# Splitting weights and tables inside the recurrence on GpSimd, and handing the first batch's rows over within the last step

## The chip, the cores and the metric

One core of one Trainium2 chip. The metric is device time in microseconds (us), the median of three runs. Engines: TensorE (PE), VectorE (DVE), ScalarE (ACT), GpSimd (POOL), and SyncE (SP), whose queue issues every DMA of this kernel.

## The reference, cut to what matters

Three layers follow each other, for 4 batches, 768 tokens and 8 heads of 40 columns (320 in all).

```
# 1 recurrence, per batch and head, over t = 0..767
y[t]  = r[t] @ state
Sa    = state @ a[t]
state = state * w[t] - outer(Sa, b[t]) + outer(v[t], k[t])
# 2 gated unit: x is y as [4, 768, 320]
h = relu(x @ w_in)                 # 320 -> 1024
g = sigmoid(conv3(h))              # three taps along the tokens
x = (h * g) @ w_out                # 1024 -> 320
# 3 Fourier mixing and a channel layer
u = x + real(fft2(x)); un = normalise(u)
out = u + relu(un @ w_ch1) @ w_ch2 # 320 -> 1280 -> 320
```

## The kernel before, in words

The kernel is two blocks of engine programs, `attention` (layer 1) and `channels` (layers 2 and 3). At the end of a block all engines meet at a barrier.

**attention.** The 768 tokens are taken in 6 steps (`STEPS`) of 128, each of two chunks of 64 (`c` = 0, 1). `attention_jobs` writes one list of jobs by hand, and each engine walks the list in that order and does its own part of each job: (stage, step g, chunk c, batch b). In step g the list does the sequential part of step g ("sat", "sa", "st", "xn", "y", "xt") beside the preparation of step g+1 (the triangular inverse by substitution, "sub", on VectorE) and of step g+2 ("scan", "at", "keys", "gram"). So a step is a column of decays (`w`) that is loaded into the tile `w_in`, scanned forward and backward on VectorE (L407, L412), and multiplied into a, k and b on GpSimd (L350, L358). GpSimd also scales the state (L365, stage "xn") and copies diagonal blocks of the inverse (L376, stage "diag"), which the jobs "pu" (TensorE, L685) wait for. SP walks the same list: it loads w for step g+1 right after the last scan of step g (L266), keys at "tb" (L280), r and v after "y" (L259, L260), and it stores y to a DRAM scratch (L318, 8 DMAs a step, rows of 128 numbers). SP is in order: each wait holds all that stands behind it.

The weights of layer 2, `w1` and `w2`, are needed in two fp32r parts, a rounded high part and the remainder. In the last step SP loads them raw (L325, five DMAs, after the last "pu"), ACT makes the high parts (L524) and VectorE the low parts (L433). SP then stores the last y and waits for all of it (L328) before the barrier.

**channels.** SP loads batch 0's rows from the DRAM scratch (L889, L891), ACT and VectorE split them (L969, L1108), and TensorE starts with `first_up` (L1291). Per batch there are 8 columns f: `first_up` (relu on ACT, L1009), the convolution (ACT L1015, VectorE L1194 and L1196), the sigmoid (ACT L1023), the gate (VectorE L1206, L1207), its split (ACT L984, VectorE L1118), and `first_down` (TensorE L1315). Then the transform (L1369 to L1384), the normalisation (L1166 to L1173), the GpSimd copy of a tail (L944), and the channel layer (L1291, L1349). From batch 1 on the channel layer of the batch before runs between these. Beside batch 0, the tables of the transform and the weights `w3` and `w4` come in 11 pieces through the tile `raw`: SP loads (L908), ACT makes the high part in `take_pieces` (L961), and GpSimd the low part (L937).

Of the kernel before, what the change touches and what calls it, by code (L numbers as in the profile page):

```python
# [19 lines left out]
DM = NH * D  # L20
# [12 lines left out]
FIRST_PIECES = 5  # L33


def attention_jobs():
# [31 lines left out]

    def kind(g, k):
        return [("gram", g, k, i) for i in range(NB)]  # L70
# [3 lines left out]
    order = each("scan", 0) + one("at", 0) + each("decays", 0) + each("keys", 0) + one("ends", 0)  # L74
# [3 lines left out]
    order += one("at", 1) + each("decays", 1) + each("keys", 1) + one("ends", 1)  # L78
    for g in range(STEPS):
        if g + 1 < STEPS:  # L80
# [15 lines left out]
            last = grams(g + 2, (1,))  # L96
            order += grams(g + 2, (0,)) + last[:2]
            order += merge(g + 1, last[2:], each("xt", g, 1, 2)) + each("decays", g + 2) + one("split", g + 2) + subs(g + 2, 0, SUBS[0])
        else:

            order += [(stage, g, 0, b) for stage in ("sat", "sa", "st") for b in range(2 if stage == "sat" else NB)]
            rest = each("xn", g, 0) + each("y", g, 0) + each("xt", g, 0, 2)
            rest += each("sat", g, 1, 2) + each("sa", g, 1) + each("st", g, 1)
            order += interleave(rest, [("table", g, 0, i) for i in range(FIRST_PIECES)])
            order += each("y", g, 1)
# [3 lines left out]
NOT_PSUM = ("scan", "at", "decays", "keys", "ends", "eye", "table", "split", "sub", "unsplit", "diag")  # L109


def first_tables(nc, ctx, dram):
# [8 lines left out]
    raw = sb("first_raw", [128, 3 * FF + NF * DM])  # L121
    pieces = []
    for t in range(3):
        cols = slice(t * FF, (t + 1) * FF)
        pieces.append((dram["w1"][:, cols], raw[:, cols], w1[:, 0, t, :], w1[:, 1, t, :]))
    n = NF * DM // 2
    parts = [w2[:, k, :, :].rearrange("p f d -> p (f d)") for k in range(2)]
    for t in range(2):
        cols = slice(t * n, (t + 1) * n)
        pieces.append((dram["w2"][:, cols], raw[:, 3 * FF + t * n:3 * FF + (t + 1) * n], parts[0][:, cols], parts[1][:, cols]))  # L130
    return w1, w2, pieces


def attention(nc, ctx, dram, tables, kept):
# [44 lines left out]
    ident, conv = kept  # L179
# [32 lines left out]

    s_piece = [sem(f"s_piece{i}") for i in range(FIRST_PIECES)]
    s_high = sem("s_high")
    s_low = sem("s_low_a")
    s_y = [sem(f"s_y{i}") for i in range(NB)]
# [33 lines left out]
    w1, w2, w_pieces = tables  # L250
# [3 lines left out]
    def _(sp):  # L254
# [6 lines left out]

        def load_w(g):
# [24 lines left out]

        load_w(0)
# [11 lines left out]
        for stage, g, c, b in order:  # L300
            more = g + 1 < STEPS
            if stage == "scan" and b == NB - 1 and more:
                load_w(g + 1)
# [1263 lines left out]
```

## Time and profile before

| what | value |
|---|---|
| median of 3 runs | 980.86 us (976.91 to 984.75) |
| profiled execution, its own time | 991.84 us |
| its span, first to last instruction | 990.0 us |
| PE busy | 860.3 us (87%) |
| DVE busy | 613.5 us (62%) |
| ACT busy | 399.6 us (40%) |
| POOL busy | 154.8 us (16%) |
| mean granted clock of TensorE | 0.924 |
| HBM read, written | 61.89 MB, 7.86 MB |

The span is the profiled execution's; it is 1.84 us less than that execution's time, and that execution was 1.1% longer than the median of the three. Busy shares are means over stages: `attention` fills the first 487 us, batch 0 of `channels` goes to about 610, and batches 1 to 3 to the end.

### The profile page before, as it was taken

The numbers are of one execution on the slowest core, as the hardware profiler recorded it, in microseconds if no ns is written. First come the engines' busy times: TensorE is split into PE (matmuls) and PEld (weight loads), VectorE is DVE, ScalarE is ACT, GpSimd is POOL, SyncE is SP. The second block draws the span as 40 slices with busy tenths as digits, with TensorE's granted clock in tenths as the row PEclk, the third lists the DMA queues.
The fourth block names the chain that finished last, engine by engine and source line by source line (L and its number), as shares of the span: only waits on it lengthen the run. The fifth ranks groups of instructions, "written<-read, shape, count | busy, mean of one in ns | idle before, by whom it ended". The sixth has DMA issues, their size and how long they took to land.

```text
span 990.0 us, 29014 instructions
## 1 busy us (share of the span) xinstructions
PE 860.3 (87%) x12628; PEld 825.4 (83%) x12628; DVE 613.5 (62%) x1167; ACT 399.6 (40%) x740; POOL 154.8 (16%) x167
## 2 busy tenths in 40 slices
PE   1648978998989989969479779999999999999998
PEld 1648877887879979869378669999999999999998
DVE  7691995875766865543379664675557663675622
ACT  1325315425426417324266324551445414552311
POOL 2015161260250440111034120000000000000000
PEclk9958997997997987979789779999999999999999
DMA  9601532461460550233322100000200002000000
GB/s 306 222 28 45 175 121 64 139 194 28 152 204 3 164 150 3 67 93 119 100 63 95 40 25 24 22 1 1 69 21 1 1 1 68 22 1 1 21 21 21
DMA packets 48847, 71.62 MB, mean 72 GB/s; under 512 B 27393, under 2 KB 38274, under 8 KB 45570
## 3 DMA queue, kind: packets, MB, share of 16 engines
q1 hardware_dynamic: 48722, 69.77, 22.7%
q8 instruction: 101, 1.65, 0.7%
q14 instruction: 24, 0.20, 0.1%
HBM read 61.89 MB, written 7.86 MB: 70 GB/s over the span
## 4 chain that ended last, share of the span: by engine, by line
PE 42%; DVE 6%; ACT 1%; issue 1%; DMA 1%; SPq 0%; DVEq 0%; POOL 0%
PE psum L1291 18%; PE psum L1349 10%; PE psum L1315 8%; PE psum L1369 2%; PE psum L1384 2%; DVE gs L1118 2%; PE psum L1282 1%; DVE cv L1196 1%; DVE cv L1194 1%; DVE gf L1206 1%; DVE res L1181 1%; DMA tok<-y_scratch 1%; PE psum L1375 0%; ACT cv L1015 0%; DVE gf L1207 0%
## 5 line engine op out<-in xcount | busy, mean ns | idle before, releaser
L1291 PE MATMUL psum<-xn,w 128*128 128x384 f32 x640 | 126.3, 340 | 3.4 <-issue 3.4
L1291 PEld LDWEIGHTS psum<-xn,w 128*128 128x128 f32 x640 | 111.5, 189 | 4.4 <-issue 4.4
L1291 PE MATMUL psum<-xs,w 128*128 128x384 f32 x512 | 97.9, 345 | 17.1 <-DVE xs L1108 14.7
L1291 PEld LDWEIGHTS psum<-xs,w 128*128 128x128 f32 x512 | 92.2, 194 | 17.6 <-DVE xs L1108 14.9
L1315 PE MATMUL psum<-w,gs 128*128 128x320 f32 x576 | 93.8, 319 | 11.1 <-DVE gs L1118 11.1
L1315 PEld LDWEIGHTS psum<-w,gs 128*128 128x128 f32 x576 | 89.5, 195 | 13.6 <-DVE gs L1118 13.6
L480 DVE TENSOR_TENSOR score<-bank,mask 128x512 f32<-128x512 f32 x48 | 32.0, 688 | 70.3 <-PE bank L710 69.9
L463 DVE TENSOR_TENSOR inv<-inv,outer 128x31 f32<-128x31 f32 (+15 forms) x186 | 64.9, 349 | 6.4
L365 POOL TENSOR_TENSOR xi<-xi,w_end 40x320 f32<-40x320 f32 x44 | 32.1, 753 | 230.2 <-issue 197.8
L461 DVE TENSOR_TENSOR outer<-low,inv 128x31 f32<-128x31 f32 (+15 forms) x186 | 62.1, 334 | 4.3
L647 PE MATMUL bank<-at,kb 64*32 64x32 f32 (+1 forms) x1536 | 31.7, 242 | 33.0 <-DVE kb L428 21.5
L1349 PE MATMUL psum<-w,hid 128*128 128x320 f32 x360 | 59.2, 310 | 1.3 <-DVE res L1181 1.3
L1194 DVE SCALAR_TENSOR_TENSOR cv<-hp,conv,cv 128x768 f32<-128x768 f32 x32 | 32.5, 1017 | 43.4 <-ACT cv L1015 43.4
L1349 PE MATMUL psum<-w,gs 128*128 128x320 f32 x360 | 59.2, 309 | 0.1
L685 PE MATMUL bank<-inv_t,rhs 128*80 128x128 f32 x384 | 56.2, 316 | 3.2 <-ACT inv_t L585 2.3
L647 PEld LDWEIGHTS bank<-at,kb 64*32 64x32 f32 x1536 | 28.6, 128 | 34.8 <-issue 34.1
L1349 PEld LDWEIGHTS psum<-w,hid 128*128 128x128 f32 x360 | 55.2, 188 | 2.0 <-issue 1.5
L1123 DVE SCALAR_TENSOR_TENSOR gs<-psum,gs 128x384 fp32r<-128x384 f32 x40 | 22.3, 557 | 55.3 <-ACT gs L994 55.3
L685 PEld LDWEIGHTS bank<-inv_t,rhs 128*80 128x80 f32 x384 | 52.9, 180 | 4.0 <-issue 3.6
L1349 PEld LDWEIGHTS psum<-w,gs 128*128 128x128 f32 x360 | 54.9, 188 | 1.2 <-DVE gs L1123 1.0
L994 ACT ACTIVATE hid<-psum 128x384 fp32r<-128x384 f32 x40 | 19.3, 490 | 81.5 <-PE psum L1291 81.5
L710 PE MATMUL bank<-rt,zt 128*128 128x128 f32 x384 | 49.6, 284 | 0.0
(137 smaller groups left out, 1711.4 us busy)
## 6 DMA issues: line engine op xcount, KB each, us to landing
kb<-in_kb SPq DMA_DIRECT2D x24, 512.0 KB, 6.3
rt<-in_rt SPq DMA_DIRECT2D x12, 1024.0 KB, 7.0
w_in<-in_w SPq DMA_DIRECT2D x6, 1040.5 KB, 5.1
at<-in_a SPq DMA_DIRECT2D x6, 1024.0 KB, 4.9
zt<-in_vt SPq DMA_DIRECT2D x12, 512.0 KB, 8.7
v_tok<-in_v SPq DMA_DIRECT2D x6, 640.0 KB, 4.1
y_scratch<-y_t SPq DMA_DIRECT2D x48, 80.0 KB
raw<-in_w SPq DMA_DIRECT2D x5, 640.0 KB, 3.8
```

Source lines behind the costliest of these rows:

```text
L365: nc.gpsimd.tensor_tensor(state, state, ends.unsqueeze(2).broadcast_to([D, NH, D]), ALU.mult).then_inc(s_x, 1)
L461: link(nc.vector.tensor_tensor(prod, low[:, b + 1:Q, b:b + 1].broadcast_to([128, n, m]), inv[:, b:b + 1, 0:m].broadcast_to([128, n, m]), A ...
L463: link(nc.vector.tensor_tensor(inv[:, b + 1:Q, 0:m], inv[:, b + 1:Q, 0:m], prod, ALU.add))
L480: nc.vector.tensor_tensor(score[:, b * NH:(b + 1) * NH, :], bank, mask[:, :].unsqueeze(1).broadcast_to([128, NH, C]), ALU.mult).then_inc(d ...
L647: last = mm(out[p:p + Q, i, 0:C - Q * q], kb[r, n, cc, 1, Q * q:Q * q + Q], at_quarters[r, n, q:2, cc, :], start=True, stop=True)
L685: last = mm(t[0:2 * D, 128 * i:128 * i + 128], rhs[:, h, :], inv_t[:, h, :, :], start=True, stop=True)
L710: last = mm(t[:, 128 * i:128 * i + 128], zt[:, c, n, :], rt[:, c, n, :, :], start=True, stop=True)
L1123: nc.vector.scalar_tensor_tensor(hid[q % 2][:, f % 2, 1, :], ps[6 + f % 2][:, 0:HALF], 0.0, f32(hid[q % 2][:, f % 2, 0, :]), ALU.max, ALU. ...
L1194: link(nc.vector.scalar_tensor_tensor(cv[:, :], h[:, 1:S + 1], conv[:, f, 1:2], cv[:, :], ALU.mult, ALU.add))
L1291: last = mm(ps[bank][:, 0:HALF], a[:, 128 * f:128 * f + 128], y[:, HALF * half:HALF * (half + 1)], start=(i == 0), stop=(i == len(every) - 1))
L1315: last = mm(ps[t][:, 0:DM], gs[:, f % 2, x, 128 * t:128 * t + 128], w2[:, y, f, :], start=(f == 0 and m == 0), stop=(f == NF - 1 and m == 2))
L1349: last = mm(ps[HALVES[k]][:, 0:DM], hid[h][:, f % 2, x, 128 * k:128 * k + 128], w4[:, y, f, :], start=(f == 0 and m == 0), stop=(f == NC - ...
```

## The change

- All weights and tables (`w1`, `w2`, `w3`, `w4` and the two transforms) lie in one DRAM array `tables` and are split inside the recurrence, in 17 pieces: 14 of 998 columns by 128 partitions and 3 of 768 columns. For each, SP loads the piece into the first half of `w_in` ("fetch"), GpSimd writes the high part into the second half and then the low part over the piece ("halve"), and SP stores both to DRAM scratch ("put"). `w_in` is idle between the last scan of a step and the first of the next. Steps 0 to 2 take three pieces each, step 3 four, step 4 the last four.
- The load of w for the next scans ("weights") moves from right behind the scans to near the step's end, behind the puts.
- In the last step the order is written out by batches: batch 0 of both chunks comes first. Its rows are loaded in two halves: the first 384 tokens at the new job "tables" near the step's start (they need no part of chunk 1 of this step), the rest at "late". ACT and VectorE split each half inside the step ("rows"). The "sa" jobs of the last chunk, whose result nobody reads, are gone.
- At "tables" SP also loads `w1` and `w2`, already split, from DRAM. The other tables are loaded, already split, at the start of `channels`, straight to their places. ACT's and GpSimd's piecewise work beside batch 0 is gone.
- The wait for the last y moves from before the barrier to the loads that need it.

```
+PIECES = [("whole", lo, min(lo + 998, WHOLE)) for lo in range(0, WHOLE, 998)]
+PIECES += [("last", lo, lo + 768) for lo in range(0, LAST_TILES, 768)]
...
-                order += interleave(second, subs(g + 1, SUBS[1], SUBS[2]))
+                if g == STEPS - 2:
+                    order += put()
+                order += fetch() + interleave(second[0:8] + halve() + second[8:], subs(g + 1, SUBS[1], SUBS[2])) + put()
             else:
-                order += first + each("st", g, 0) + kind(1, 1) + one("split", 1)
+                order += first + halve() + each("st", g, 0) + kind(1, 1) + put() + one("weights", 2) + one("split", 1)
...
+            order += fetch()
             order += one("at", g + 2)
...
-            third += each("st", g, 1) + keys[2:4] + each("xn", g, 1)
-            order += interleave(third, subs(g + 1, SUBS[2], SUBS[3])) + one("ends", g + 2)
-            order += interleave(each("y", g, 1), subs(g + 1, SUBS[3], SUBS[4])) + one("unsplit", g + 1) + one("eye", g + 2)
+            third += each("st", g, 1) + keys[2:4] + halve() + each("xn", g, 1)
+            order += interleave(third, subs(g + 1, SUBS[2], SUBS[3])) + one("ends", g + 2) + put() + fetch()
+            order += interleave(each("y", g, 1) + halve(), subs(g + 1, SUBS[3], SUBS[4])) + one("unsplit", g + 1) + one("eye", g + 2)
             last = grams(g + 2, (1,))
-            order += grams(g + 2, (0,)) + last[:2]
-            order += merge(g + 1, last[2:], each("xt", g, 1, 2)) + each("decays", g + 2) + one("split", g + 2) + subs(g + 2, 0, SUBS[0])
+            order += grams(g + 2, (0,)) + last[:2] + put()
+            if g < STEPS - 3:
+                order += one("weights", g + 3)
+            else:
+                order += fetch()
+            order += merge(g + 1, last[2:], each("xt", g, 1, 2)) + (halve() if g >= STEPS - 3 else []) + each("decays", g + 2) + one("split", g + 2) + subs(g + 2, 0, SUBS[0])
...
+            order += put() + sat[0][0:1] + sat[0][1:2] + one("tables", g) + sa[0][0:2] + st[0][0:2] + sa[0][2:4] + xn[0][0:2]
+            order += st[0][2:4] + y[0][0:2] + xt[0:1] + sat[1][0:1] + xn[0][2:4] + st[1][0:2] + y[0][2:3] + y[1][0:1]
+            order += one("rows", g) + y[0][3:4] + xt[1:2] + sat[1][1:2] + y[1][1:2] + st[1][2:4] + y[1][2:3] + [("late", g, 0, 1)]
+            order += y[1][3:4] + [("rows", g, 0, 1)]
...
+            if stage == "fetch":
+                sp.wait_ge(s_decay, NB * scanned)
+                if b:
+                    sp.wait_ge(s_put, 32 * b)
+                table, lo, hi, x, high = piece(b)
+                sp.dma_start(x, dram["tables"][:, lo + (WHOLE if table == "last" else 0):hi + (WHOLE if table == "last" else 0)]
+                             ).then_inc(s_fetch, 16)
+            if stage == "put":
+                table, lo, hi, x, high = piece(b)
+                sp.wait_ge(s_phigh, b + 1)
+                if table == "whole":
+                    sp.dma_start(dram["high"][:, lo:hi], high.bitcast(F32)).then_inc(s_put, 16)
+                    sp.wait_ge(s_plow, b + 1)
+                    sp.dma_start(dram["low"][:, lo:hi], x).then_inc(s_put, 16)
...
+            if halved[0]:
+                sp.wait_ge(s_put, 32 * halved[0])
             sp.dma_start(w_in[:, :], dram["w"][g]).then_inc(s_w, 16)
...
+            if stage == "tables":
...
+                load_rows(0)
+                sp.wait_ge(s_put, 32 * len(PIECES))
+                for k, part in enumerate(("high", "low")):
+                    sp.dma_start(w1[:, k, 0:2, :].rearrange("p t f -> p (t f)").bitcast(F32), dram[part][:, 0:W1]).then_inc(s_w1, 16)
+                sp.dma_start(w1[:, 0, 2, :].bitcast(F32), dram["last"][:, 0:FF]).then_inc(s_w1, 16)
+                for k, part in enumerate(("high", "low")):
+                    sp.dma_start(w2[:, k, :, :].rearrange("p f d -> p (f d)").bitcast(F32), dram[part][:, W1:W1 + W2]).then_inc(s_w2, 16)
+            if stage == "late":
+                load_rows(1)
...
+            elif stage == "halve":
+                table, lo, hi, x, high = piece(b)
+                pool.wait_ge(s_fetch, 16 * (b + 1))
+                nc.gpsimd.tensor_copy(high, x).then_inc(s_phigh, 1)
+                pool.wait_ge(s_phigh, b + 1)
+                nc.gpsimd.tensor_tensor(x.bitcast(F32R), x, high.bitcast(F32), ALU.subtract).then_inc(s_plow, 1)
...
+            elif stage == "rows":
+                cols = slice(HALF * b, HALF * b + HALF)
+                dve.wait_ge(s_x0hi, b + 1)
+                nc.vector.tensor_tensor(xs[:, 1, :, cols], x_in[:, :, cols], xs[:, 0, :, cols].bitcast(F32),
+                                        ALU.subtract).then_inc(s_x0, 1)
```

## Rows read from the trace of the kernel before

**Rows 1.** Busy time by stage: stretch, length, busy us (count) of each engine, PEclk, DMA share, GB/s

```profile
264.00:336.00 72.00, 66.56 (x1691) 62.43 (x1690) 51.15 (x107) 30.14 (x63) 21.09 (x20) 0.91 0.42 130
453.00:481.00 28.00, 26.67 (x564) 25.65 (x562) 15.64 (x22) 12.27 (x21) 4.11 (x4) 1.00 0.31 106
496.00:556.00 60.00, 48.74 (x258) 46.84 (x258) 48.53 (x42) 37.51 (x51) 23.09 (x10) 0.89 0.27 82
```

**Rows 2.** The last work of the recurrence: VectorE in order of time

```profile
481.07 1.42 DVE L495 TENSOR_TENSOR y_t<-bank,y_t 128x256 f32<-128x256 f32 x4
```

**Rows 3.** The chain that ended last, at the handover: start, us, what

```profile
487.23 0.39 SPq L889
...
488.23 5.58 DMA tok<-y_scratch
...
493.83 0.84 ACT xs L969
...
495.71 5.50 PE psum L1291 x16
```

**Rows 4.** The same chain, further on: batch 0, and a full-clock column of batch 1

```profile
555.35 4.28 PE psum L1315 x18
...
628.87 2.79 PE psum L1291 x16
631.67 2.63 PE psum L1315 x18
```

**Rows 5.** VectorE in order of time, batch 0

```profile
511.14 2.41 DVE L1206 TENSOR_TENSOR gf<-hp,sg 128x385 f32<-128x385 f32 x1
...
527.53 3.68 DVE L1118 TENSOR_TENSOR gs<-gf,gs 128x768 fp32r<-128x768 f32 x1
...
574.59 1.22 DVE L1166 COPY res<-half_row 1x320 f32<-1x320 f32 x1
```

**Rows 6.** GpSimd in order of time, batch 0

```profile
527.48 2.92 POOL L937 TENSOR_TENSOR w<-raw,w 128x1280 fp32r<-128x1280 f32 x1 [4.67 <-ACT w L961]
```

**Rows 7.** One line's instructions, all batches: duration ns min/median/max

```profile
L1118 DVE TENSOR_TENSOR gs<-gf,gs x32: 950/953/3693, 510.1 to 887.7; 128x768 fp32r<-128x768 f32 x32
```

**Rows 8.** Groups of GpSimd by line and shape: count, busy us, mean ns, idle before

```profile
L376 POOL COPY inv_t<-inv_d 32x1024 f32<-32x1024 f32 x12 | 13.9, 1159 | 73.1 <-DVE inv_d L475 56.6 <-issue 16.2
L937 POOL TENSOR_TENSOR dft_s<-raw,dft_s 128x1158 fp32r<-128x1158 f32 x2 | 6.0, 3003 | 19.8 <-ACT dft_s L961 19.8
```

**Rows 9.** GpSimd in order of time, steps 2 and 3

```profile
264.43 2.78 POOL L365 TENSOR_TENSOR xi<-xi,w_end 40x320 f32<-40x320 f32 x4 [44.22 <-issue]
...
284.60 2.78 POOL L365 TENSOR_TENSOR xi<-xi,w_end 40x320 f32<-40x320 f32 x4
290.68 2.13 POOL L376 COPY inv_t<-inv_d 32x1024 f32<-32x1024 f32 x2 [3.31 <-issue]
...
343.14 6.89 POOL L358 TENSOR_TENSOR kb<-kb,after 128x512 f32<-128x512 f32 x6
```

**Rows 10.** VectorE in order of time, step 3

```profile
343.39 0.38 DVE L461 TENSOR_TENSOR outer<-low,inv 128x220 f32<-128x220 f32 x1
```

**Rows 11.** SP's DMA issues in order of time, step 2

```profile
263.94 0.33 SPq L266 DMA_DIRECT2D w_in<-in_w  x1
...
284.85 2.46 SPq L318 DMA_DIRECT2D y_scratch<-y_t  x6
```

**Rows 12.** TensorE in order of time, step 2

```profile
294.68 0.42 PE L647 MATMUL bank<-at,kb 64*32 64x64 f32 x6 [4.72 <-issue]
...
307.79 3.38 PE L685 MATMUL bank<-inv_t,rhs 128*80 128x128 f32 x16
```

**Rows 13.** Busy time in stretches of 2 us, step 2, columns as in Rows 1

```profile
290.00:292.00 2.00, 0.00 (x0) 0.00 (x0) 1.68 (x3) 1.35 (x3) 1.26 (x2) 1.00 0.98 384
...
296.00:298.00 2.00, 2.00 (x50) 2.00 (x48) 0.69 (x1) 0.00 (x0) 0.00 (x0) 0.50 0.04 8
```

**Rows 14.** Busy time in a stretch of 4 us, step 2, columns as in Rows 1

```profile
264.00:268.00 4.00, 4.00 (x102) 3.50 (x101) 3.83 (x10) 0.79 (x2) 3.57 (x5) 1.00 0.96 330
```

More of the change, by code:

```diff
@@ L72, in attention_jobs @@
     SUBS = (16, 16, 21, 29, Q - 1)
-    order = each("scan", 0) + one("at", 0) + each("decays", 0) + each("keys", 0) + one("ends", 0)
+    order = each("scan", 0) + one("weights", 1) + one("at", 0) + each("decays", 0) + each("keys", 0) + one("ends", 0)
     order += kind(0, 1) + one("eye", 0) + one("split", 0)
@@ L77, in attention_jobs @@
     order += one("unsplit", 0) + one("eye", 1) + merge(0, [], []) + each("scan", 1)
-    order += one("at", 1) + each("decays", 1) + each("keys", 1) + one("ends", 1)
+    order += one("at", 1) + each("decays", 1) + each("keys", 1) + one("ends", 1) + fetch()
     for g in range(STEPS):
@@ L106, in attention_jobs @@
     return order
-NOT_PSUM = ("scan", "at", "decays", "keys", "ends", "eye", "table", "split", "sub", "unsplit", "diag")
+NOT_PSUM = ("weights", "fetch", "halve", "put", "tables", "rows", "late", "scan", "at", "decays", "keys", "ends", "eye", "split", "sub", "unsplit", "diag")
 def first_tables(nc, ctx, dram):
@@ L120, in first_tables @@
     w2 = sb("w2", [128, 2, NF, DM], F32R)
[L121 to L131, printed above, removed]
+    xs = sb("xs", [128, 2, 3, S], F32R)
+    tok = sb("tok", [128, NT, 384])
+    return w1, w2, xs, tok
 def attention(nc, ctx, dram, tables, kept):
@@ L211, in attention @@
     s_x = sem("s_x")
[L213 to L216, printed above, removed]
+    s_fetch = sem("s_fetch")
+    s_phigh = sem("s_phigh")
+    s_plow = sem("s_plow")
+    s_put = sem("s_put")
+    s_xin = sem("s_xin")
+    s_x0hi = sem("s_x0hi")
     def kb_slot(g, c):
@@ L248, in attention, with piece @@
     inv_1, merged = inner[0:2 * Q], inner[2 * Q:4 * Q]
-    w1, w2, w_pieces = tables
+    w1, w2, xs, tok = tables
+    x_in = tok[:, :, :].rearrange("p t d -> p (t d)").rearrange("p (k s) -> p k s", k=3)
+    def piece(i):
+        table, lo, hi = PIECES[i]
+        n = hi - lo
+        return table, lo, hi, w_in[:, 0:n], w_in[:, n:2 * n].bitcast(F32R)
     block = ctx.enter_context(nc.Block())
@@ L301, in _ @@
             more = g + 1 < STEPS
-            if stage == "scan" and b == NB - 1 and more:
-                load_w(g + 1)
+            if stage == "weights":
+                load_w(g)
+            if stage == "fetch":
[12 more added lines that the diff above has]
+                    sp.dma_start(dram["low"][:, lo:hi], x).then_inc(s_put, 16)
+                else:
+                    sp.dma_start(dram["last"][0:64, lo:hi], high[0:64].bitcast(F32)).then_inc(s_put, 16)
+                    sp.wait_ge(s_plow, b + 1)
+                    sp.dma_start(dram["last"][64:128, lo:hi], x[64:128]).then_inc(s_put, 16)
+                halved[0] += 1
+            if stage == "scan":
+                scanned = g + 1
             if stage == "ta" and b == NB - 1 and more:
@@ L954, in _ @@
     def _(act):
[L955 to L962 removed]
         def rows_high(b, k):
[L965 to L968 removed]
+            act.wait_ge(s_yin, 48 * b)
+            act.wait_ge(s_spec, 4 * b)
             nc.scalar.copy(xs[:, 0, k, :], x_in[:, k, :]).then_inc(s_xhi, 1)
@@ L994, in hidden_high @@
             nc.scalar.activation(hid[q % 2][:, f % 2, 0, :], ps[6 + f % 2][:, 0:HALF], ACT.Relu).then_inc(s_hhi, 1)
-        for k in range(3):
-            rows_high(0, k)
+        act.wait_ge(s_odd_in, 16)
+        nc.scalar.copy(odd[:, :], odd_in[:, :]).then_inc(s_odd, 1)
         for b in range(NB):
@@ L1045, in spectrum_high @@
                 nc.scalar.copy(ef[:, 0, i, dt, :], ps[SPECTRUM[i, dt]][:, 0:NP]).then_inc(s_fhi, 1)
+            if b == 0:
+                for i in range(1, NB):
+                    act.wait_ge(s_y[i], 32 * STEPS)
             for i in range(NT):
@@ L1559 @@
     dram["y"] = nc.dram_tensor("y_scratch", (NB, DM, S), F32, kind="Internal").ap()
+    for name, columns in (("high", WHOLE), ("low", WHOLE), ("last", LAST_TILES)):
+        dram[name] = nc.dram_tensor(f"{name}_scratch", (128, columns), F32, kind="Internal").ap()
     dram["out"] = nc.dram_tensor("out", (NB, NT, 128, DM), F32, kind="ExternalOutput").ap()
```

174 lines of the change are left out of this document (76 added, 98 removed).

## The prediction

> **What bounds the kernel now.** I read the busy time by stage first. The reader is to see that TensorE is the bound nearly everywhere: 66.6 of 72 us in a step of the recurrence and 26.7 of 28 in the last step [rows 1], and in batch 1 its groups of matmuls follow each other without a gap, 628.87 + 2.79 to 631.67 [rows 4]. Two places are not like this. Batch 0's first stage has TensorE busy for 48.7 of 60 us [rows 1]. And between the two blocks TensorE does nothing: VectorE drains the last y until 482.5 [rows 2], SP starts to read it back at 487.2, the data land at 493.8, ACT and VectorE split a third of it, and the first matmul starts at 495.71 [rows 3], some 14.7 us after the last matmul of the recurrence at about 481. The change aims at both, and puts work into the recurrence, where TensorE has 5.4 us to spare in 72.
>
> Then I read the single engines in order of time where TensorE waits. In batch 0 VectorE's low part of a gate takes 0.95 us in the median and 3.68 us at 527.53 [rows 5, 7]; GpSimd's low part of a table piece ran from 527.48 to 530.40 [rows 6]. VectorE's instruction ended 0.8 us after GpSimd's, so it did its work only then. Seven such instructions on the gate's lines are stretched in the stage, from the one at 511.14 (2.41 us, where the shape takes 0.56) to one at 549.84; their excess sums to 15.2 us.
>
> The Trainium skill, SBUF — State Buffer, "SBUF: two separate sides", says that VectorE and GpSimd share a pair of ports under an exclusive lock, which a VectorE instruction needs if it reads two SBUF operands or runs in a two-port mode, and that the loser blocks for the whole instruction. By that rule, the trace agrees (3.68 against 0.95).
>
> **The handover.** Last step: before, 453.3 to 481.0. The new order keeps the jobs, drops the last four "sa" (32 short transposes, some 1.8 us of TensorE), and ACT's and VectorE's splitting of w1 and w2. I walked the new order with one job each of sat 1.05, sa 0.45, st 0.92, xn 0.65, y 0.94, xt 0.6 us (a 28 us stage with 26.7 busy [rows 1], divided by its jobs) and found no wait that isn't covered by the neighbouring batch pair; TensorE ends at about 479.5. The last load of rows stands behind three of the four y stores of chunk 1; I put its issue at 480.8. It carries half the rows: 5.58 us for all of them [rows 3], so 3.5 us taken for half, landing at 484.3. ACT takes 0.84 us for 768 columns [rows 3], so 1.2 for 1152; VectorE 0.97 for 768, so 1.4. That is 487.0; the barrier adds 0.5 and the first matmul stands at 487.7. Gain 8.0 us. Bounds: nothing hidden of the load and a y store more in front, gain 5; a load as fast as half of 5.58, gain 9. The waits that SP now carries in front ("tables" for the last put, then 5 DMAs of 5.2 MB of split weights instead of 2.9 MB) end long before: issued at about 455, at the 330 GB/s of a burst [rows 14] they are in by 472. ACT and VectorE wait inside their queues for the rows; behind them stand only the barrier's arrivals.
>
> **Batch 0.** From the first matmul to the last `first_down` it now takes 495.71 to 555.35, 59.6 us [rows 3, 4]. Without GpSimd's pieces VectorE's stretches go, and with ACT's copies gone (0.7 to 1.3 us each, eleven) the loop ACT sigmoid 0.85, relu 0.85, ACT tap 0.94, VectorE taps 2.05 is 4.7 us a column. TensorE needs 2.79 + 2.63 = 5.42 us a column [rows 4], so TensorE is next late. Filling: the first column at the half clock 5.5 us [rows 3], then 9.4 us of that chain until its first `first_down`; then five columns of 5.42 (27.1); then the last column's chain relu to low part 7.3 us. 14.9 + 27.1 + 7.3 = 49.3. Gain 10.3; I take 9.5, as some waits won't overlap so well. Ends: 5 (half of the stretches sit where TensorE had work anyway, since it idled only 11.3 us in the stage [rows 1]), and 11.3.
>
> After the transform the copy at 574.59 took 1.22 us [rows 5] where the same copy takes 0.32 in batch 1, and the tail copy on GpSimd came late by 0.4: gain 1.3. The new loads of 10 MB at the start of `channels` need some 31 us at 330 GB/s, while the first of them is used 54 us in: nothing. If that cover were gone it would show as a TensorE wait before the transform.
>
> **The recurrence.** Seventeen halvings. GpSimd's copy of 1024 columns takes 1.06 us undisturbed (2.13 for two [rows 9]; the group's mean is 1.16), a subtraction of 1158 columns 3.0 [rows 8], so 998 columns take 2.3 to 2.6: 3.5 us each, 60 us of GpSimd in all. GpSimd is busy for 21 of 72 us in a step [rows 1]; three more halvings make 31.5. Nobody but VectorE could feel it, and the substitution beside GpSimd's products keeps its 0.38 us [rows 9, 10], since one operand is in PSUM. The scans read SBUF twice, but the order ends the scans before a fetch. So the occupancy costs nothing; the order might. Behind the first halving of a step stand "at" and "keys", behind the second the state's scaling (284.60), behind the third the diagonal copy (290.68) [rows 9]. Walking step 2: fetch at 264 instead of w [rows 11], landed 268, halved 271.5; keys end at 284.8 against 284.6, because they waited for their data before; put 276, landed 281.5, fetch landed 285.7, halved 289.1; scaling done 291.9 against 287.4, its reader ("xt") is at 306; put landed 292.5, fetch landed 296, halved 299.4, diagonal done 301.5 against 292.8. Its reader is L685 at 307.79 [rows 12]: 6 us of room. In step 0 there is none, for its third fetch lands some 4 us later: 0 to 3 us.
>
> SP is the other queue. The y stores and the load of r and v for chunk 1, at 284.85 [rows 11], now stand behind the second put, and move to about 293. Before, this burst stops TensorE: the last 6 of 128 equal matmuls come 4.72 us late with no wait shown [rows 12], inside one job, while the DMA engines are at 0.98 [rows 13]; behind it the clock is 0.50, its lower level of 1.2 GHz, against 1.00 [rows 13]. I count five such gaps of 3.5 to 4.8 us, one a step after the first. I read them as the instruction stream starved by the burst. Moved by 8 us, the burst still meets short 32-row matmuls (mj, gram, mt), so I keep the gap. What is new is its length: 1.5 MB of pieces and 1.04 MB of w join it. I charge 3 us for the recurrence in all. Ends: −8 (w no longer loads beside the keys, and a gap falls where TensorE waits anyway) and +25 (each gap half as long again, with the half clock behind it, 5 us in five steps).
>
> The Trainium skill, Runtime: NRT & Kernel Launch, "Instruction fetch mechanics", says that an engine's instructions are refilled by a DMA queue of its own and that this is mostly hidden. By it the gaps have another cause and the recurrence term is 0, not 3; the 4.72 us inside one job speaks against it.
>
> **The sum.** −8.0 − 9.5 − 1.3 + 3.0 = −15.8. The profiled execution's 991.84 becomes 976.0. From the median of 980.86, which ran the same program 1.1% faster, I take the same difference: 965 us.
>
> **The rivals.**
> - *Starved TensorE (slower).* Each of the five steps from 0 on gets a second gap, because puts, fetches and the late w keep the DMA engines full through the short matmuls. A gap costs 4.7 us and 8 us at half clock behind it, another 4: 9 × 5 = 45, less 19 gained, gives 1007. It decides from 19 + 10 us, that is one more gap in three steps. Against it: with w and the keys in flight the DMA engines are at 0.96 from 264 to 268, and TensorE is busy for all 4 us [rows 14]. Chance 0.11.
> - *GpSimd's queue becomes the bound.* Put and fetch land slower than I took (a store's landing isn't shown alone), the diagonal copy passes 307.8 and "pu" waits. 3 us past it in each of four steps is 12, with the 3: 977. For it: two round trips of DRAM per halving in line. Chance 0.16.
> - *The gains are hidden.* The barrier stays late and batch 0 turns on ACT: 5 + 5 + 1.3 − 3 = 8: 972.5. Chance 0.10.
> - *The gaps go.* Moved, the burst falls where TensorE has its instructions: 4 × 7 more gained, 937. Chance 0.11.
>
> **Chances.** My forecast has 0.52, with its own range 956 to 974. A change under 1% either way (971 to 990.7) is what a measurement here can't tell from none. Faster: 0.47 of mine, 0.11, 0.05 of the hidden gains, and 0.06 of the GpSimd case: about 0.70. Slower 0.11. Same 0.19. For 8 in 10 the range leaves out the starved case and the lowest end of the last one: 942 to 987.
>
> **What would show it.** First `first_up` 14.7 us after the last matmul becomes 7 to 9; L1118 and L1206 at 0.95 and 0.56 throughout; first stage of batch 0 near 50 us; the diagonal copy 6 us before the first L685 in steps 1 to 3; y stores some 8 us later in the step; one TensorE gap a step, no longer than 7 us. I am wrong if a step of the recurrence, 72 us, grows by more than 3.

## The result, and the profile after

The changed kernel took 976.4 us in the median (966.41 to 983.3, 20 runs) beside 983.08 us before (972.91 to 990.99, 20 runs): ratio 0.9935, 95% interval [0.991, 0.9961], 6.7 us less. Ratios leave out executions that are over 1.5% above the fastest of the same kernel. It was measured twice more beside other kernels: 0.9949 [0.9913, 0.9986] and 0.9936 [0.9901, 0.997]. The forecast was 15.8 us less. The profiled execution went from 991.84 to 977.17 us, 14.7 less, which looks like the forecast and misleads, as will be seen.

Busy time by stage of the changed kernel: step 2, the last step, batch 0's first stage; columns as in [rows 1].

```profile
265.00:340.00 75.00, 66.56 (x1674) 62.07 (x1672) 51.21 (x106) 30.37 (x63) 29.88 (x26) 0.91 0.59 182
456.00:484.00 28.00, 25.89 (x520) 24.75 (x514) 11.70 (x20) 6.05 (x11) 2.81 (x4) 0.94 0.62 230
493.00:543.00 50.00, 45.74 (x260) 44.42 (x259) 31.56 (x40) 29.23 (x43) 0.50 (x2) 0.92 0.50 206
```

Against [rows 1] batch 0's stage is 10 us shorter and TensorE idles 4 us in it instead of 11. But a step of the recurrence has 75 us instead of 72 with the same 66.56 us of TensorE work, and its DMA share went from 0.42 to 0.59.

The handover, which answers to [rows 2, 3], in order of time on SP, ACT, VectorE and TensorE:

```profile
484.56 0.62 SPq L323 DMA_DIRECT2D tok<-y_scratch  x1
489.11 1.15 ACT L592 CAST xs<-tok 128x1152 fp32r<-128x1152 f32 x1 [9.82 <-DMA tok<-y_scratch]
490.29 1.36 DVE L508 TENSOR_TENSOR xs<-tok,xs 128x1152 fp32r<-128x1152 f32 x1 [5.65 <-ACT xs L592]
492.13 1.30 PE L1326 MATMUL psum<-xs,w 128*128 128x384 f32 x3 [7.95 <-PEq L1521]
```

TensorE's idle time between the blocks is 7.95 us, where it was 14.7. The half load takes 4.5 us from issue to landing, ACT 1.15 and VectorE 1.36.

Batch 0 in the chain that ended last, answering to [rows 4], and the copy of [rows 5] in VectorE's order of time:

```profile
492.13 5.32 PE psum L1326 x16
...
542.71 0.80 ACT res L1077 x2
...
567.07 3.44 issue
570.51 2.90 PE psum L1326 x8
```

```profile
560.27 0.32 DVE L1207 COPY res<-half_row 1x320 f32<-1x320 f32 x1
```

And the two lines of VectorE whose stretched instructions [rows 5, 7] showed, all batches: duration min/median/max.

```profile
L1159 DVE TENSOR_TENSOR gs<-gf,gs x32: 949/951/961, 505.7 to 872.7; 128x768 fp32r<-128x768 f32 x32
```

```profile
L1245 DVE TENSOR_TENSOR gf<-hp,sg x32: 560/562/565, 502.0 to 870.8; 128x385 f32<-128x385 f32 x32
```

No instruction is stretched any more: 3693 has become 961 ns, and 2.41 us [rows 5] 0.565.

The recurrence. TensorE's longest waits in step 2, in the order of time, which answer to the one gap of [rows 12], then one of step 4 and one of the last step ("issue" is time in which the engine waits for nothing that the view names):

```profile
287.92 0.25 PE L798 MATMUL bank<-score,kb_tok 128*40 128x64 f32 x1 [1.91 <-issue]
...
296.93 0.30 PE L715 MATMUL bank<-at,kb 64*32 64x64 f32 x6 [1.65 <-issue]
...
305.25 1.06 PE L715 MATMUL bank<-at,kb 64*32 64x32 f32 x48 [2.39 <-issue]
...
310.48 0.53 PE L742 MATMUL bank<-inv_d,inner 32*32 32x32 f32 x12 [1.90 <-issue]
...
444.37 3.67 PE L753 MATMUL bank<-inv_t,rhs 128*80 128x128 f32 x16 [4.82 <-POOL inv_t L452]
...
475.60 0.25 PE L798 MATMUL bank<-score,kb_tok 128*40 128x64 f32 x2 [2.11 <-issue]
```

One gap of 4.72 us has become four of 1.6 to 2.4. Two waits are new in kind. In step 4 TensorE waits for the diagonal copy. In the last step a gap stands in the sequential part, and the clock behind it is half (477 to 479 us):

```profile
477.00:479.00 2.00, 2.00 (x44) 2.00 (x42) 0.00 (x0) 0.51 (x2) 0.00 (x0) 0.50 0.04 8
```

What the "issue" gaps are can be read from the kept traces. Beside the queue of the kernel's own transfers, the profile of either kernel lists a DMA queue q8 of the kind "instruction", with 101 packets and 1.65 MB. Its packets are 16 KB each, and the trace has the time of each. Number TensorE's records (weight loads, matmuls and its semaphore events) by their start: in step 2 the ones behind the four gaps are 11457, 11969, 12481 and 12737, which are 256 or twice 256 apart, and 11969 also stands behind the one gap of [rows 12]. These gaps end 1.3 to 1.6 us after a packet landed (286.42, 295.61, 303.84 and 308.88 us). The 20 kept profiles have 268 idle times of TensorE over 1 us between 93 us and the end of the recurrence that stand at such a place, one of every 256 records; each ends 1.1 to 1.7 us after a landing. All others over 1 us there wait for VectorE or GpSimd. In the kernel before, TensorE passed the place ahead of the gap of 4.72 us at 287.74, and the next packet started only at 292.18, 4.44 us later, while the DMA engines were at 0.98 [rows 13]; behind the gap the next one started after 1.36 us. So TensorE stands because the packet with its next instructions comes late behind the data.

GpSimd in order of time, steps 2 and 4: a halving is 1.01 + 1.95 us, and the diagonal copy stands behind the third one.

```profile
302.65 1.95 POOL L434 TENSOR_TENSOR w_in<-w_in 128x998 fp32r<-128x998 f32 x1
304.55 2.12 POOL L452 COPY inv_t<-inv_d 32x1024 f32<-32x1024 f32 x2
...
442.00 2.12 POOL L452 COPY inv_t<-inv_d 32x1024 f32<-32x1024 f32 x2
```

In step 2 it ends at 306.7, 6.1 us before its reader at 312.79; in step 4 it ends at 444.12, and the reader starts at 444.37.

Since one profiled execution can mislead, I read the same marks from all of them (us; each mark is the start or the end of one instruction in the order of time). "pu" is the end of the last copy of pu before the last step, "up" the first `first_up`, "kept" the first tile that ACT takes after batch 0's first stage, "second" the first `second_up` of the channel layer.

| kernel | pu | pu to up | up to kept | kept to second | second to end |
|---|---|---|---|---|---|
| before | 454.0 | 41.7 | 60.4 | 30.1 | 403.8 |
| before again | 453.3 | 41.0 | 60.3 | 30.1 | 403.9 |
| changed | 455.7 | 36.4 | 50.6 | 27.8 | 404.9 |
| changed again | 464.3 | 34.6 | 50.4 | 31.0 | 405.2 |
| changed, third | 459.2 | 33.1 | 49.7 | 27.6 | 404.7 |

By the means of these rows the change is worth −6.7 (handover), −10.1 (batch 0), −1.3 (behind it), +1.1 (the rest) and +6.1 us (recurrence), in sum −10.9. The timed runs say some −6. What is behind the recurrence repeats within 1 us, but for the handover (3.3 us) and the 31.0 from kept to second in one execution; the recurrence scatters by 9 us between executions of one kernel. Both profiled executions of before (991.84 and 990.38 us) lie above the medians of the timed ones beside them (983.1 and 985.0).

### The profile page after: what moved, and what is told of

It is laid out like the page before. It is cut to its first block, busy times and chain, and to the rows that moved or that the text cites. A ratio compares the mean times of both kernels' runs of the same rounds, so it can differ in the third digit from the quotient of the medians.

```text
span 975.4 us, 29043 instructions
## 1 busy us (share of the span) xinstructions
PE 856.5 (88%) x12612; PEld 821.6 (84%) x12612; DVE 589.9 (60%) x1159; ACT 383.6 (39%) x720; POOL 175.1 (18%) x191
## 3 DMA queue, kind: packets, MB, share of 16 engines
q8 instruction: 101, 1.65, 0.7%
## 4 chain that ended last, share of the span: by engine, by line
PE 44%; DVE 4%; ACT 1%; issue 1%; DVEq 0%; POOL 0%; ACTq 0%
PE psum L1326 20%; PE psum L1386 11%; PE psum L1352 8%; PE psum L1406 2%; PE psum L1421 2%; PE psum L1317 1%; DVE cv L1235 1%; DVE cv L1233 1%; DVE res L1222 1%; DVE gs L1159 1%; PE psum L1412 0%; ACT cv L1058 0%; DVE tok L1180 0%; ACT hp L1052 0%; DVE stats L1212 0%
## 5 line engine op out<-in xcount | busy, mean ns | idle before, releaser
L1352 PE MATMUL psum<-w,gs 128*128 128x320 f32 x576 | 90.1, 310 | 4.2 <-DVE gs L1159 4.1
L1352 PEld LDWEIGHTS psum<-w,gs 128*128 128x128 f32 x576 | 86.4, 188 | 6.2 <-DVE gs L1159 6.2
L552 DVE TENSOR_TENSOR score<-bank,mask 128x512 f32<-128x512 f32 x48 | 32.4, 688 | 69.8 <-PE bank L778 69.0
L1386 PE MATMUL psum<-w,gs 128*128 128x320 f32 x360 | 59.6, 310 | 0.0
L1386 PEld LDWEIGHTS psum<-w,gs 128*128 128x128 f32 x360 | 55.4, 188 | 1.1 <-DVE gs L1164 1.0
L798 PE MATMUL bank<-score,kb_tok 128*40 128x64 f32 x768 | 47.6, 223 | 5.9 <-issue 5.9
```

The source lines that it names most:

```text
L552: nc.vector.tensor_tensor(score[:, b * NH:(b + 1) * NH, :], bank, mask[:, :].unsqueeze(1).broadcast_to([128, NH, C]), ALU.mult).then_inc(d ...
L798: last = mm(o, kb_tok[:, kb_slot(g, c), 2 * n + k, :], score[:, 2 * n + k, :], start=False, stop=True)
L1352: last = mm(ps[t][:, 0:DM], gs[:, f % 2, x, 128 * t:128 * t + 128], w2[:, y, f, :], start=(f == 0 and m == 0), stop=(f == NF - 1 and m == 2))
L1386: last = mm(ps[HALVES[k]][:, 0:DM], hid[h][:, f % 2, x, 128 * k:128 * k + 128], w4[:, y, f, :], start=(f == 0 and m == 0), stop=(f == NC - ...
```

## The experiments

Ratios are to the kernel before, with 95% intervals. In the runs that leave a part of the split out, `w1` to `w4` and the transforms are filled from pieces that exist, by loads of the same size, so that everything behind the recurrence stays as it is; their output isn't the reference's. The transfers alone and the stores alone load what they stored.

**The changed kernel, and the kernel before, again.** No edit.

> The changed kernel once more, as the yardstick of this set. Both theories: 0.9935 of before within 0.003. Stages as in its first profile: first matmul of the second block some 8 us after the last of the recurrence, batch 0's first stage near 50 us. Where the two theories differ is the recurrence: theory 'recurrence' says the steps before the last end at 455 or later, since the split costs 10 us or more there in a typical execution; theory 'gains' says the recurrence costs about 3 us as I charged and the gains behind it are smaller in a typical execution.

> The kernel before once more, for a second trace: how much of the profiled pair's 14.6 us is chance in the recurrence. Both theories: batch 0's first stage again 60 us from first matmul to first kept tile, and 13 us from the last y to the first matmul; last copy of pu at 450 to 454.

Measured: 979.01 us, 0.9949 [0.9913, 0.9986]; the profiled execution of before 990.38 us. Their marks are in the table above. A profile of the changed kernel lies 3.1 to 15.8 us below one of the kernel before, by which pair one takes, so a single pair doesn't price the change.

**Without the split.**

```
-    return order
+    return [j for j in order if j[0] not in ("fetch", "halve", "put") or j[3] == 0]
```

> The changed kernel without the split in the recurrence: only the first of the 17 pieces is fetched, halved and put; all later loads of weights and tables read that piece over and over, so the output isn't the reference's. The load of w, the last step's order and the handover stay. Theory 'recurrence': the split costs some 11 us, so this gains 18 to 19 us on before (0.981) and 11 on the changed kernel. Theory 'gains': it gains 3 us on the changed kernel (0.990).

> The kernel without the split once more, to have its time with a narrow interval beside the three above: only the first piece is fetched, halved and stored, and the tables are later loaded from it over and over, so the output is not the reference's. If traffic is the split's price, 0.985 to 0.989 (the changed kernel had 0.9935 and 0.9949); if its first measurement was only the luck of few runs, 0.993 or more.

Measured: 0.9875 [0.9821, 0.9929], and again 0.9879 [0.9827, 0.993]. The changed kernel has 0.9935, 0.9949 and 0.9936. So the split costs the recurrence 0.006 of 983, about 6 us; without it the change would be worth 12.

**The old last step, with and without the split.** The order of before's last step and its loads of rows in `channels` are back; the second run leaves the split out as well, and so has batch 0's gain alone.

```
+            order += put() + one("tables", g)
+            order += [(stage, g, 0, b) for stage in ("sat", "sa", "st") for b in range(2 if stage == "sat" else NB)]
+            order += each("xn", g, 0) + each("y", g, 0) + each("xt", g, 0, 2)
...
-                load_rows(0)
```

> The changed kernel with the last step in the old order (four more sa jobs) and with batch 0's rows loaded and split behind the barrier, as before; the presplit weights are still loaded in the last step. My sum gave the handover 8.0 us: then this is 8 us slower than the changed kernel, 1.001 of before. If the new last step loses part of it to its own waits, the difference is 2 to 5 us.

> Both edits together: old last step and no split in the recurrence (output not the reference's, as in e2). What is left of the change is batch 0 without the pieces on ACT and GpSimd, and no splitting of w1 and w2 in the last step. My terms: 9.5 + 1.3 = 10.8 us, 0.989 of before. Theory 'gains' says 5 us, 0.995.

Measured: 0.9996 [0.9968, 1.0025] with the split, 0.9926 [0.9892, 0.996] without it. Against the changed kernel and the kernel without the split, the new last step is worth some 5 us both times, the forecast's lower bound. With the split but without the new last step, the change would be worth nothing.

**The transfers alone, and GpSimd's work alone.** The first line is the one's, the second the other's; waits that lose their other side wait for the transfer or the halving that is left.

```
+    return [j for j in order if j[0] != "halve"] 
...
+    return [j for j in order if j[0] not in ("fetch", "put") or j[3] == 0]
```

> The changed kernel with all 17 fetches and puts but without the halvings on GpSimd; SP waits for the fetch's landing instead, and stores the second half of w_in as it is (output not the reference's). In the set before, three executions with the split ended the step before the last (last copy of pu) at 455.7, 464.3 and 460.5 us, two without it at 451.4 and 449.7. Theory 'traffic': the cost of some 10 us is the DMA engines' load, which starves TensorE's instruction stream in several small gaps; then this kernel ends it at 457 to 460 and stands at 0.991 of before. Theory 'queue': the cost is GpSimd's order (the diagonal copy behind a halving that waits for its fetch, 4.8 us seen before pu in step 4); then this ends it near 452, and the kernel stands at 0.983.

> The halvings alone: all 17 on GpSimd at their places in the order, but only the first piece is fetched and put, so no halving waits for a DMA; later loads read that piece over and over (output not the reference's). Both theories expect little: GpSimd's 50 us lie in its idle time, VectorE's operands are in PSUM. Last copy of pu near 451, time within 2 us of the kernel without the split, 0.9875 of before or less. If the occupancy itself costs, 455 to 458.

Measured: transfers alone 1.0044 [1.0007, 1.0082], GpSimd alone 0.9921 [0.9891, 0.9952]. The busy time from 90 to 450 us, columns as in [rows 1]: before,

```profile
90.00:450.00 360.00, 319.52 (x8126) 298.54 (x8125) 243.27 (x513) 142.48 (x298) 91.97 (x90) 0.90 0.36 107
```

GpSimd alone,

```profile
90.00:450.00 360.00, 320.09 (x8120) 299.13 (x8119) 242.27 (x512) 143.21 (x299) 139.19 (x123) 0.89 0.38 113
```

and the transfers alone:

```profile
90.00:450.00 360.00, 312.97 (x7911) 291.31 (x7910) 241.84 (x512) 135.45 (x285) 91.07 (x90) 0.88 0.51 160
```

GpSimd's 47 us more leave TensorE as it was (320.09 busy, as many matmuls as before). The transfers cost TensorE 6.6 us of the 360 and some 215 matmuls of progress, without one halving on GpSimd. GpSimd alone lies 4 us above no split, with intervals that overlap; the tiny pieces below, with all of GpSimd's work, are level with no split.

**The diagonal copy first.** The third piece is halved and stored behind the diagonal copy, and the y stores stand ahead of the second put.

```
-            order += interleave(each("y", g, 1) + halve(), subs(g + 1, SUBS[3], SUBS[4])) + ...
+            order += interleave(each("y", g, 1), subs(g + 1, SUBS[3], SUBS[4])) + put() + fetch() + ...
...
+            order += merge(g + 1, last[2:], each("xt", g, 1, 2)) + halve() + put()
```

> The changed kernel with another order in steps 0 to 4, all work kept: the second put and third fetch stand behind the y stores on SP (the stores go back to some 285 us in step 2), and the third halving and put behind the diagonal copy and the pu jobs. Theory 'queue': the 4.8 us before pu in step 4 go, and up to 1 us in step 3: 5 us faster than the changed kernel, 0.989. Theory 'traffic': the bytes are the same and only move, so 0 to 2 us, unless they leave the short matmuls; then as much as 8. Against both: w now lands last, some 4 us before its scan; if it comes late, VectorE waits on it at the step's start and the time is that of the changed kernel or worse.

Measured: 0.9942 [0.9906, 0.9979], as the changed kernel. The wait of 4.82 us for the diagonal copy is gone, and in its place stands what before had there too (4.66 at 438.09), TensorE in order of time:

```profile
444.36 0.58 PE L734 MATMUL bank<-inner,gram_m 32*32 32x32 f32 x14 [4.39 <-issue]
```

This matmul is record 18625, one of the places where a packet of instructions is due, and stands some 200 records ahead of the one that waited for GpSimd. So the wait had not covered this gap: the order that takes away the one brings back the other, and the time stays. What the wait costs by itself isn't shown.

**Fetches alone, stores alone, stores doubled.** In this order:

```
+    return [j for j in order if j[0] not in ("halve", "put") or j[3] == 0]
...
+    return [j for j in order if j[0] not in ("fetch", "halve") or j[3] == 0]
...
+                for again in ("", "_2"):
+                        sp.dma_start(dram["high" + again][:, lo:hi], high.bitcast(F32)).then_inc(s_put, 16)
```

> As the changed kernel, but of the pieces behind the first only the 16 fetches are left (8.5 MB read from DRAM into w_in); their halvings on GpSimd and their stores are left out, and the tables are later loaded from the first piece over and over, so the output is not the reference's. If the split costs the recurrence by the bytes that it moves, a third of them is here: some 3 us more than without any split, a ratio of 0.990 to 0.992 to the kernel before, and the last pu of the recurrence near 454 us. If it costs by the two stores and the wait for their landing on SP's queue, the fetches are free: 0.9875 to 0.989, last pu near 451.

> As the changed kernel, but behind the first piece the 16 fetches and halvings are left out and only the 32 stores stay (17 MB written; what they write is whatever w_in holds, so the output is not the reference's). By the bytes: two thirds of the cost, 5 to 7 us more than without a split, ratio 0.993 to 0.996, last pu near 458. If a read that shares the DMA engines with the loads is what hurts, and stores are cheap: 0.988 to 0.990.

> The changed kernel with each store of a piece issued twice, the second time to a scratch of its own: 17 MB more written, all results as in the changed kernel. By the bytes: the split's price of 8 to 10 us grows by two thirds, ratio 1.000 to 1.003, last pu near 464, and several TensorE gaps a step. If only the place of the diagonal copy and of the y stores behind the puts mattered, they would pass the first pu by far more in steps 1 to 3: waits of TensorE on GpSimd's inv_t of 3 us or more in each step, ratio 1.01 and over. If bytes don't matter: 0.994 as the changed kernel.

Measured: 0.9967 [0.9934, 1.0], 1.0004 [0.9969, 1.0038] and 1.0149 [1.009, 1.0208]. Against no split that is 9, 12 and 27 us. TensorE in order of time, stores doubled:

```profile
165.68 2.60 PE L754 MATMUL bank<-inv_t,rhs 128*80 128x128 f32 x11 [2.70 <-POOL inv_t L453]
...
240.18 3.67 PE L754 MATMUL bank<-inv_t,rhs 128*80 128x128 f32 x16 [2.66 <-POOL inv_t L453]
...
317.10 1.11 PE L754 MATMUL bank<-inv_t,rhs 128*80 128x128 f32 x4 [1.40 <-POOL inv_t L453]
...
459.53 2.82 PE L754 MATMUL bank<-inv_t,rhs 128*80 128x128 f32 x12 [8.29 <-POOL inv_t L453]
```

Here the forecast's rival, GpSimd's queue as the bound, has come true: 15.1 us of waits for the diagonal copy in four steps. In the three profiles of the changed kernel they are 5.4, 4.9 and 5.2. But fetches alone and stores alone each cost more than both with the halvings between them (6 us), and neither has such a wait. Bytes alone don't order these runs.

**By place: without the third piece of a step, and the third alone** (pieces 0, 2, 5, 8, 11, 15).

```
+    kept = [0, 1, 3, 4, 6, 7, 9, 10, 12, 13, 14, 16]
+    return [(j[0], 0, 0, kept.index(j[3])) if j[0] in moves else j for j in order if j[0] not in moves or j[3] in kept]
```

> The changed kernel without the third piece of each step (5 of 17 pieces gone: their fetch, halving and stores, all of which lie in the stretch of short matmuls and beside the y stores); the tables are later loaded from the first piece over and over, so the output is not the reference's. If what counts is bytes, wherever they go, 12 of 17 pieces keep 70% of the price of 6 us: ratio 0.992. If it is the third piece's place, in front of the y stores, the diagonal copy and the short matmuls, nearly all of the price goes: 0.988 to 0.989, and the wait of TensorE for inv_t in step 4 (4.82 us) is gone.

> The changed kernel with the first piece and the third piece of each step alone (6 of 17); the other 11 are left out, and the tables are loaded from the first piece over and over, so the output is not the reference's. By bytes: 0.989 to 0.990. By the third piece's place: 0.992 to 0.994, as the whole change.

> The changed kernel again, beside the two above, so that the three share their runs of the kernel before: 0.994, as in its two measurements, under any theory.

Measured: 1.0012 [0.9982, 1.0043], 0.9941 [0.9902, 0.9979] and 0.9936 [0.9901, 0.997]. The first run failed both theories: with five pieces fewer the kernel is slower than with all 17. The third piece alone has the time of the whole change, as the theory of its place has it. This could have been SP: without the third piece's waits nothing holds the y stores, r, v and w back from the put in front of them.

**The waits without the bytes.** Every job stays, but a piece moves 16 columns: all pieces behind the first, or each step's third (2, 5, 8, 11, 15).

```
+        if i in range(1, len(PIECES)):
+            return table, lo, lo + 16, x[:, 0:16], high[:, 0:16]
```

> The changed kernel with every wait, DMA and halving in its place, but each piece behind the first moves 16 columns in place of 998 (768), so that SP's queue keeps its order and its waits while the bytes are nearly gone; the tables are later loaded from the first piece over and over, so the output is not the reference's. If the split's price is the bytes: 0.986 to 0.989, as without a split. If it is SP's waits and what they hold back (w, y stores, r and v): 0.993 or more.

> The changed kernel, but only the third piece of each step moves 16 columns; all waits and the other twelve pieces stay (tables loaded from the first piece over and over, output not the reference's). It has the bytes of the run that left the third pieces out (1.0012) and the queue order of the changed kernel. If that run was slow because SP, freed of the third piece's waits, issued w, r, v and the y stores earlier into the other pieces: 0.988 to 0.992 here. If it was slow by the two pieces' own bytes: 0.999 or more.

> The kernel without the third piece of each step once more (output not the reference's), beside the two above. If its 1.0012 is a property of this order of transfers, 0.998 to 1.004; if it was chance between chips, about 0.992.

Measured: 0.9883 [0.9833, 0.9932], 0.991 [0.9877, 0.9944] and 0.9976 [0.9935, 1.0016]. With all of SP's waits, 48 tiny transfers and GpSimd's halvings, but without the bytes, the price is nothing (no split: 0.9875 and 0.9879). A tiny transfer also lands sooner, so the waits are kept but shorter. The busy time of that kernel,

```profile
90.00:450.00 360.00, 325.09 (x8185) 304.08 (x8186) 242.10 (x512) 145.56 (x303) 139.33 (x123) 0.88 0.39 114
```

beside the changed kernel's:

```profile
90.00:450.00 360.00, 316.93 (x8095) 295.12 (x8094) 242.74 (x512) 141.38 (x295) 137.43 (x122) 0.90 0.55 173
```

TensorE idles 43 us in this stretch instead of 35, at 173 GB/s instead of 114: 5.4 us more are the wait for the diagonal copy, which is gone with tiny pieces, and 2.7 more are "issue" (32.8 beside 30.1). So the price is the traffic, by both ways. With the third piece's waits and order kept and its bytes gone, 12 pieces cost 3 us; with its waits gone too, 9 and 13 (the second run, 0.9976, overlaps with the changed kernel's intervals). From record 2600 to 19000 of TensorE, the same work in all, the idle time where packets of instructions are due is 27.0 us with the tiny third piece and 39.7 and 35.8 without it; it is 32.9, 35.7 and 34.5 in the changed kernel, 43.7 in the transfers alone, 29.6 with all pieces tiny, 32.4 and 29.2 without the split, 34.1 and 30.9 in the kernel before. The three dearest of these (13, 9 and 16 us against no split) are those in which TensorE stands longest for its instructions. What differs is SP's order, step 2, DMA issues in order of time. Without the third piece, its second run:

```profile
296.50 0.32 SPq L366 DMA_DIRECT2D low_scratch<-w_in  x1
296.92 4.02 SPq L388 DMA_DIRECT2D y_scratch<-y_t  x6
...
306.17 1.28 SPq L307 DMA_DIRECT2D w_in<-in_w  x1
```

With the tiny one:

```profile
289.95 0.32 SPq L370 DMA_DIRECT2D low_scratch<-w_in  x1
293.69 0.33 SPq L362 DMA_DIRECT2D w_in<-in_tables  x1
294.12 3.37 SPq L392 DMA_DIRECT2D y_scratch<-y_t  x6
```

The tiny fetch waits 3.4 us for the store's landing, and only then do the y stores, r and v follow; without it the y stores are issued 0.1 us behind the store. That is the difference in these rows. There is another: the 12 pieces that are left are numbered anew, so all are whole ones, and that kernel writes 20.13 MB where the one with the tiny pieces writes 18.94, about 1.4 MB more with the reads. That is little for the 6 to 10 us between them, since the whole split moves 22 MB for its 6 us. That the lost wait is the cause is argued, not shown.

## Why the prediction was wrong

**What bounds the kernel: right.** TensorE idled in batch 0's stage and at the handover, and these are where the gain came from.

**The handover, −8.0 (5 to 9): right in kind, at the lower part of its bounds.** The idle time is 7.95 us, in the forecast's 7 to 9; ACT's 1.15 (1.2), VectorE's 1.36 (1.4) and the barrier's 0.48 (0.5) are as worked out, and the half load took 4.5 us to land instead of 3.5. (The forecast's own terms, 480.8 + 3.5 + 1.2 + 1.4 + 0.5, make 487.4 and not 487.7.) What didn't come in this execution is the 1.5 us from the last step itself: it ends its y at 484.6, 28.9 us after pu (before 28.5 and 27.9); the gap of 2.11 us and the half clock behind it stand there. In the two other executions of the changed kernel the last step takes 26.4 and 25.9 us, so there it came. From pu to the first matmul it is 6.7 us in the mean, by the timed runs 5.

**Batch 0, −9.5 (5 to 11.3): right.** 60.4 became 50.2 us in the mean, forecast 49.3. The Trainium skill, SBUF — State Buffer, "SBUF: two separate sides", had VectorE blocked by GpSimd's instruction; with GpSimd's subtractions gone from the stage the longest of 32 is 961 ns, so the trace after agrees too. In the recurrence 17 subtractions of GpSimd stretch nothing: no VectorE instruction of the changed kernel from 85 to 450 us takes over 1.3 times the median of its line and shape, and with tiny pieces the halvings cost nothing by the timed runs.

**The copy and the tail, −1.3: right**, 1.22 to 0.32 us for the copy and 1.3 us by the marks in the mean. The new loads of 10 MB are not quite free: from the first `second_up` to the end 1.1 us more, which the forecast didn't have, and in one of the three executions the stage from kept to second didn't shrink (31.0).

**GpSimd's occupancy, 0: right.** 3.0 us a piece (3.5 taken), the diagonal copy 6.1 us ahead of its reader in step 2 (6). But in step 4, which the walk didn't go through, it came too late.

**The recurrence, +3.0 (−8 to +25): this term failed, by its size.** The mechanism was right, an instruction stream held up by the burst. I charged 3 us because "1.5 MB of pieces and 1.04 MB of w join" the burst, as if each step had one gap that only grows. The profiles give +6.1, the timed runs more: −6 is −17 (the other four terms) plus the recurrence, so +11, if the other terms are in a timed run what they are in the profiled ones, which is so but for the handover. 6 of these 11 are the traffic of the split, by the runs that keep the waits and drop the bytes. The 5 others are in every kernel that has no split traffic as well (0.9875 to 0.9883 where −17 would be 0.983; 0.9926 for batch 0 alone, where its terms with 1.8 us at the handover make 0.988). They may be the place of w's load, which all of them share, or before's two profiled executions may not be typical of the stages behind the recurrence. This wasn't tried and stays open.

The forecast expected one longer gap a step, "no longer than 7 us". What came is more and smaller ones, with TensorE idle for 43 us of 360 instead of 35 to 40, and a step that grew from 71.7 to 74.7 us between the ends of its scans (81.3 in the second execution, 74.7 in the third). My own condition, "grows by more than 3", was met by 6 us in the second execution; the other two stand at its edge. The y stores moved by 13.3 us, not 8: 284.85 [rows 11] to 298.18, of which 2.2 us are the later start of the step.

**The sum.** "I take the same difference" from a median 1.1% below the profiled execution was the second failure. The profiled execution was forecast as 976.0 and came as 977.17, but the base was at the top of the spread. The excess seems to lie in the recurrence, where the change adds, and not in the stages that it shortens: those differ by 0.7 us at most between before's two profiles. No profile of before near its median shows it, so this is argued.

**The rivals.** *Starved TensorE* was the right mechanism with a wrong price: in steps 1 and 2 of the first profile four gaps come in place of one, but each is 1.5 to 2.7 us (3.8 at most in the second profile), in step 3 two of 1.3 and 1.5, and in step 4 none; doubling the stores moves the kernel to 15 us above before, towards this rival's case. *GpSimd's queue becomes the bound* came in part: step 4 waits in the first two profiles of the changed kernel (4.82 and 4.90 us), two steps (2.66 and 2.51 us) in the third, and four with doubled stores. *The gaps go* didn't happen. The rule from Runtime: NRT & Kernel Launch, "Instruction fetch mechanics" in the Trainium skill, that refills have a DMA queue of their own and are mostly hidden, holds in its first half (q8 above) and not in its second: from record 2600 to 19000, 27 to 44 us of idle time stand at the refills, and the recurrence term is not 0 but 6 us of traffic at least. The prediction took the rule for one that gives the gaps another cause; the packets show that refills are their cause.

## What to carry to other kernels

Work moved to an idle engine can be free while the transfers that carry it there are not: price the bytes by an experiment that keeps the waits and moves 16 columns. TensorE's next 256 instructions come through the same DMA engines as the data. Long matmuls hide this, short ones don't: in the changed kernel 256 records with long matmuls last 8.5 us (318.74 to 327.25); in the short ones a packet started 1.35 us after TensorE went on at 296.93 and still held it up for 0.52 us before 300.60, and any delay adds to that. Letting one burst land before the next is issued went with more gain here than moving fewer bytes: the transfers alone move as many bytes as the changed kernel and are 10 us slower. Before a gain is carried from a profile to a median, see whether what made that execution long lies in the stages that the change touches.

## What the runs showed that I had not expected

Fewer transfers were slower: 12 pieces 1.0012 and 0.9976, 17 pieces 0.9936 to 0.9949; and fetches and stores without the halvings between them 1.0044, with them 0.994. I read this as GpSimd's instructions pacing the transfers. And most of TensorE's idle time in the recurrence, 34 of 40 us in the kernel before, is a wait for its own instructions, which the views only call "issue"; a gap that ends at every 256th record, just behind an instruction packet, is its sign.
